# A mixture-of-experts kernel: the loads of an expert's weights issued one block later on ACT, with flags for the blocks around in the table of experts

## The chip, the cores and the metric

The kernel runs on one core of a Trainium2 chip. The time is the device time of one execution in microseconds, and lower is better. Five engines work side by side, each with an instruction queue of its own: PE (matrix products), ACT and DVE (element-wise work), POOL (here mostly gathers and scatters by index) and SP (here only DMAs). They wait for each other by semaphores.

## The reference

Three stages follow each other. Shapes: q, k, v and alpha are 4 x 8 x 768 x 48, which gives 3072 tokens of 384 features.

```python
for t in range(S):                       # gated linear attention
    state = alpha[:, :, t, :, None] * state + einsum('bhd,bhe->bhde', k[:, :, t], v[:, :, t])
    y[:, :, t] = einsum('bhd,bhde->bhe', q[:, :, t], state)
# mixture of 8 experts, one per token: w1 is (8, 384, 1024), w2 is (8, 1024, 384)
expert_idx = argmax(normalised(x) @ normalised(expert_emb).T / tau, axis=1)
for e in range(8):
    mask = expert_idx == e
    h = maximum(x[mask] @ w1[e], 0.0)
    out[mask] = gate_w[mask, None] * (h @ w2[e])
# last network: w_in is (384, 2048), w_out is (2048, 384)
h = x @ w_in
return maximum(0.01 * h, h) @ w_out
```

## The kernel before

Products are made in parts: each fp32 operand is split into a rounded part, which ACT writes, and the rest, which DVE gets by subtracting that from the original; three products of parts replace one. So every weight is loaded as fp32 into `raw`, rounded by ACT (`split_hi`, L409) and subtracted by DVE (`split_lo`, L415) into `wts`. `wts` has two sets; expert e uses set e & 1. `raw` has a half for w1 and a half for w2, each 1.5 MB, which takes three DMAs (`load_half`, L423), three roundings and three subtractions ("pieces"). A half of `raw` can be loaded again once DVE has subtracted its three pieces, for which `load_half` waits on its engine (`w_lo[half]`).

The experts' stage (about 137 to 450 us of the execution) works on 31 windows of 128 tokens, sorted by expert, at most one expert a window. The table `wtab` holds for each window its expert and a flag for the first window of an expert. With these inputs experts 0 to 7 have 4, 3, 3, 4, 4, 3, 3 and 7 windows (the last are partly empty), so windows 0, 4, 7, 10, 14, 18, 21 and 24 are first ones.

Each engine runs `step(w, u)` for w = 0 to 30, u being w's parity. In order:

- PE: x·w1 of window w + 2 (`block_hidden`, L1519, 18 matmuls), in an odd window with the transposes of h of window w between its halves (`turn_h`, L1530); the transposes of the rows of window w + 3 (`turn_gx`, L1495); then h·w2 of window w (`contract`, L1539, 24 matmuls).
- ACT: the two halves of h of window w rounded into `hT` (`h_round`: L816 from PSUM in odd windows, L820 from `hds` in even ones); relu of window w + 2 (L805, L810); the rounding of the rows of window w + 3 (`gx_round`, L799); if w + 2 is the first window of an expert, the next expert's w1 rounded and then the w1 after that loaded (`first_weights`); if w is a first window, the same with w2 (`second_weights`).
- DVE: the rests of these, in the same order (L1268 or L1271 for hT, L1142 for the rows, L415 for the weights), and last the copy of window w's result out of PSUM (L1315), for which the next contraction and POOL's scatter wait.
- In even windows h is turned by DVE in 32 x 32 squares (L1261) and SP moves the squares to their place by 16 small DMAs (`move_h`, L531, hds<-hs), for which ACT's L820 waits. POOL gathers the rows of window w + 4 (L652).

The order on each engine is written by hand; windows 4 to 27 or so are the body of a hardware loop, of two windows. ACT's part of the step that is concerned ends so:

```python
if ahead(w, 2):
    e, first = follower(act, w + 2)
    with act.If(first > 0):
        first_weights(w + 2, e)
e, first = follower(act, w)
with act.If(first > 0):
    second_weights(w, e)
```

Of the kernel before, what the change touches and what calls it, by code (L numbers as in the profile page):

```python
# [24 lines left out]
def build(nc, qka, v, emb, tau, weights, x_dram, y_dram, gate_dram, out):  # L25
# [9 lines left out]
    E, F = weights.shape[0] - 2, 1024  # L35
# [39 lines left out]
    with ExitStack() as ctx:  # L75
# [307 lines left out]
        def table(eng, w):  # L383

            return eng.value_load(wtab[0:1, ds(w, 1)], min_val=0, max_val=2 * E - 1)  # L385
# [45 lines left out]
        def next_expert(eng, e):  # L431
            return e + 1 if isinstance(e, int) else eng.snap(e + 1)

        def follower(eng, w):

            code = table(eng, w)
            return eng.snap((code & (E - 1)) + 1), eng.snap(code & E)
# [269 lines left out]
        def _(act):  # L707
# [145 lines left out]
            def step(w, u):  # L853
                if isinstance(w, int) and w == 0:

                    e, first = follower(act, 1)
                    with act.If(first > 0):
                        first_weights(0, 1)
                        first_weights(1, e)
# [5 lines left out]
                    with act.If(act.snap(E - first) > 0):  # L865
# [14 lines left out]
                with act.If(first > 0):  # L880
                    second_weights(w, e)
# [10 lines left out]
            each_window(act, step)  # L892
# [44 lines left out]
        def _(dve):  # L937
# [217 lines left out]
            start("main", dve.scalar_tensor_tensor(out=code, in0=first, scalar=float(E), in1=expert, op0=ALU.mult, op1=ALU.add))  # L1155
            after("main")
# [117 lines left out]
            def step(w, u):  # L1274
                if isinstance(w, int) and w == 0:
                    e, first = follower(dve, 1)
                    with dve.If(first > 0):
                        split_lo(dve, 1, 1, W1_PIECES)
                        split_lo(dve, e, next_set(dve, e), W1_PIECES)
                    gx_rest(2, 0)  # L1280
                    place_slots()
                for half in range(2):
                    h_rest(w, u, half)
                if isinstance(w, int) and w == 0:
                    with dve.If(dve.snap(E - first) > 0):
                        split_lo(dve, 1, 1, W1_PIECES)
# [8 lines left out]
                if ahead(w, 2):  # L1295
                    e, first = follower(dve, w + 2)
                    with dve.If(first > 0):
                        split_lo(dve, e, next_set(dve, e), W1_PIECES)
                e, first = follower(dve, w)
                with dve.If(first > 0):  # L1300
                    split_lo(dve, e, next_set(dve, e), W2_PIECES)
# [405 lines left out]
```

## Time and profile before

| | |
|---|---|
| median of 3 runs | 851.62 us (851.6 to 852.6) |
| the profiled execution's own time | 852.63 us |
| its span in the profile | 850.9 us |
| PE busy | 819.3 us, 96% of the span |
| PE weight loads, DVE, ACT, POOL busy | 86%, 51%, 40%, 24% |
| mean granted clock of PE | 0.996 |
| chain that ended last | PE 80%, DVE 5%, issue 5%, ACTq 3%, ACT 3% |

The profiled execution is the slowest of the three. Its span leaves out 1.7 us of the time. The busy share of PE is that of matmuls that overlap, so that it says little of what could be gained; the waits ahead of its matmuls say more.

### The profile page before, as it was taken

To read this page: it belongs to the slowest core of one execution; us is meant where nothing else is said; L and a number is where in the kernel's file an instruction comes from. 1 tells how busy PE (TensorE), PEld (TensorE's weight loads), DVE (VectorE), ACT (ScalarE), POOL (GpSimd) and SP (SyncE) were. 2 spreads that over 40 slices of the span, in tenths; PEclk is the share of its full clock that TensorE was granted. 3 is DMA by queue.
4 is the path that set the end of the run, shared out by engine and by line. 5 is a ranking of instruction groups with operands and counts; after the bars stand their busy time and mean duration, and the time that the engine had idled before them with its cause. 6 is when DMAs were issued, how large, how long until landed. Compare 5 with 4: busy or idle time off the path is not lost.

```text
span 850.9 us, 17254 instructions
## 1 busy us (share of the span) xinstructions
PE 819.3 (96%) x5379; PEld 734.0 (86%) x5380; DVE 434.1 (51%) x672; ACT 341.9 (40%) x643; POOL 200.0 (24%) x279
## 2 busy tenths in 40 slices
PE   7999999899989999899999999999999999999998
PEld 6888887788878888788998998998998988898997
DVE  7899986656455454455265433533433443343332
ACT  2555564444344443444253323333333333333233
POOL 6667613122233222323124003003002001000100
PEclk9999999999999999999999999999999999999999
DMA  9988665644464446647303201201011000000101
GB/s 222 268 250 245 190 205 183 204 137 129 134 219 142 142 140 169 216 158 190 101 4 41 38 1 38 37 1 37 6 32 37 1 0 18 19 1 0 38 1 38
DMA packets 55384, 85.83 MB, mean 101 GB/s; under 512 B 26855, under 2 KB 40723, under 8 KB 55344
## 3 DMA queue, kind: packets, MB, share of 16 engines
q1 hardware_dynamic: 39248, 45.24, 19.9%
q10 hardware_dynamic: 10208, 25.23, 9.0%
q0 software_dynamic: 5888, 14.85, 5.3%
q8 instruction: 22, 0.36, 0.2%
q14 instruction: 18, 0.15, 0.1%
HBM read 63.69 MB, written 15.64 MB: 93 GB/s over the span
## 4 chain that ended last, share of the span: by engine, by line
PE 80%; DVE 5%; issue 5%; ACTq 3%; ACT 3%; DMA 1%; POOL 1%; DVEq 0%; SPq 0%; POOLq 0%
PE bank L1566 24%; PE bank L1611 24%; PE bank L1539 11%; PE bank L1519 9%; PE bank L1361 2%; PE bank L1401 2%; DVE wts L415 2%; PE bank L1378 2%; ACT wts L409 2%; ACTq L423 2%; PE bank L1409 1%; PE bank L1367 1%; PE bank L1530 1%; ACTq L385 1%; PE bank L1421 1%
## 5 line engine op out<-in xcount | busy, mean ns | idle before, releaser
L1566 PE MATMUL bank<-yT,wts 128*128 128x512 f32 x864 | 217.3, 395 | 0.9 <-DVE ys L1315 0.9
L1611 PE MATMUL bank<-wts,gs 128*128 128x384 f32 x1152 | 215.4, 335 | 0.4 <-ACT os L910 0.2
L1611 PEld LDWEIGHTS bank<-wts,gs 128*128 128x128 f32 x1152 | 202.2, 188 | 10.6 <-issue 1.6
L1566 PEld LDWEIGHTS bank<-yT,wts 128*128 128x128 f32 x864 | 160.6, 188 | 31.9 <-issue 1.2
L1185 DVE TENSOR_TENSOR g<-bank,small 128x512 f32<-128x512 f32 x96 | 66.4, 691 | 175.7 <-ACT small L847 175.7
L1539 PE MATMUL bank<-wts,hT 128*128 x744 | 138.5, 341 | 17.0 <-DVE hT L1268 8.7
L1539 PEld LDWEIGHTS bank<-wts,hT 128*128 128x128 f32 x744 | 129.6, 190 | 20.7 <-issue 20.5
L1519 PE MATMUL bank<-wts,gxT 128*128 (+1 forms) x549 | 134.9, 395 | 1.3 <-DVE gxT L1142 1.3
L847 ACT ACTIVATE small<-bank 128x512 f32<-128x512 f32 x96 | 57.6, 600 | 186.5 <-PE bank L1566 186.0
L1519 PEld LDWEIGHTS bank<-wts,gxT 128*128 128x128 f32 x549 | 101.3, 188 | 20.8 <-issue 1.6
L1328 DVE TENSOR_TENSOR gs<-g,gs 128x512 fp32r<-128x512 f32 x96 | 66.5, 693 | 66.4 <-ACT gs L921 66.4
L921 ACT ACTIVATE gs<-g 128x512 fp32r<-128x512 f32 x96 | 60.7, 632 | 77.6 <-DVE g L1185 74.6
L701 POOL DMA_INDIRECT out<-os,tokens x20 | 19.7, 986 | 288.1 <-ACT os L910 283.5
L415 DVE TENSOR_TENSOR wts<-raw,wts 128x1024 f32 (+1 forms) x60 | 70.2, 1220 | 21.4 <-ACT wts L409 20.9
L678 POOL DMA_INDIRECT y_rows<-ys,idst x31 | 33.5, 1081 | 201.3 <-DVE ys L1315 193.6
L409 ACT ACTIVATE wts<-raw 128x1024 f32 (+1 forms) x60 | 59.5, 1055 | 11.2 <-issue 10.8
L816 ACT ACTIVATE hT<-bank 128x512 fp32r<-128x512 f32 x34 | 18.5, 595 | 66.4 <-issue 37.3
L820 ACT ACTIVATE hT<-hds 128x512 fp32r<-128x512 f32 x28 | 16.1, 624 | 57.7 <-DMA hds<-hs 21.6
L1315 DVE COPY ys<-bank 128x384 f32<-128x384 f32 x31 | 17.1, 553 | 43.1 <-PE bank L1539 43.1
L1268 DVE TENSOR_TENSOR hT<-bank,hT 128x512 fp32r<-128x512 f32 x34 | 21.9, 685 | 33.5 <-ACT hT L816 33.5
L652 POOL DMA_INDIRECT xg<-x_rows,isrc x27 | 29.6, 1095 | 23.8 <-POOL isrc L647 23.8
L605 POOL TENSOR_TENSOR qt<-qkas,decay 112x512 f32<-112x512 f32 x24 | 30.7, 1280 | 17.5 <-DVE decay L960 17.5
(174 smaller groups left out, 762.6 us busy)
## 6 DMA issues: line engine op xcount, KB each, us to landing
raw<-weights ACTq DMA_DIRECT2D x48, 512.0 KB
qkas<-qka SPq DMA_DIRECT2D x20, 675.5 KB, 5.7
hds<-hs SPq DMA_DIRECT2D x224, 32.0 KB
raw<-weights SPq DMA_DIRECT2D x12, 512.0 KB
vs<-v SPq DMA_DIRECT2D x24, 192.0 KB, 4.6
x_rows<-xs SPq DMA_DIRECT2D x24, 192.0 KB, 3.8
yl<-y_rows SPq DMA_DIRECT2D x20, 192.0 KB, 5.1
qkas<-qka SPq DMA_DIRECT2D x4, 227.5 KB, 6.8
```

What stands on the lines that cost most here:

```text
L409: act.activation(set_of(par, 0, cols), raw[:, cols], ACT.Copy).then_inc(w_hi[j // 3], 1)
L415: dve.tensor_tensor(set_of(par, 1, cols), raw[:, cols], set_of(par, 0, cols).bitcast(F32), ALU.subtract).then_inc(w_lo[j // 3], 1)
L605: pool.tensor_tensor(qt[0:PW, b], q_in[b][0:PW], decay[0:PW, b], ALU.mult).then_inc(qt_ready, 1)
L678: pool.indirect_dma_start(out=y_dram, out_offset=bass.IndirectOffsetOnAxis(ap=idst[:, u:u + 1].bitcast(U32), axis=0), in_=ys[:, u, :], in_ ...
L847: act.activation(small[:, f % 2], gps[f % 2][:, :], ACT.Copy, scale=0.01).then_inc(small_done, 1)
L921: act.activation(gs[:, f % 4, 0], g[:, f % 2], ACT.Copy).then_inc(g_hi, 1)
L1185: dve.tensor_tensor(g[:, f % 2], gps[f % 2][:, :], small[:, f % 2], ALU.max).then_inc(g_done, 1)
L1328: dve.tensor_tensor(gs[:, f % 4, 1], g[:, f % 2], gs[:, f % 4, 0].bitcast(F32), ALU.subtract).then_inc(g_lo, 1)
L1519: m = pe.matmul(hps[u][half][:, :], gxT[:, u, x_part, k * P:(k + 1) * P], set_of(par, w_part, slice(n, n + HALF)), start=(k == 0 and (x_pa ...
L1539: m = pe.matmul(yeps, hT[:, h_part, k * P:(k + 1) * P], set_of(par, w_part, slice(n, n + D)), start=(k == 0 and (h_part, w_part) == (0, 0) ...
L1566: m = pe.matmul(gps[f % 2][:, :], wts[:, 0, w_part, n:n + P], yT[:, 1 - u, y_part, k], start=(k == 0 and (w_part, y_part) == (0, 0)), stop ...
L1611: m = pe.matmul(ops[tt], gs[:, f % 4, g_part, tt * P:(tt + 1) * P], wts[:, 1, w_part, f * D:(f + 1) * D], start=(f == 0 and (g_part, w_par ...
```

## The change

`load_half` leaves `first_weights` and `second_weights`. ACT now issues the load of w1 in the window after that of the roundings which it follows, and that of w2 likewise, right behind `gx_round`. To know when, the table gets three more flags per window (is w + 1, w + 2 or w - 1 the first window of an expert), made by three more operations of DVE, and ACT and DVE read the table at the head of each step (`experts`), ACT once more for each load. The roundings of expert 1's w2 move from window 0 to window 1, and the load behind them to window 2. ACT's windows 2 and 3 are written out ahead of the loop. PE's, POOL's and SP's programs stay.

The diff, ACT's step first, then DVE's table and, last, DVE's step:

```diff
-        def follower(eng, w):
+        def experts(eng, w):
             code = table(eng, w)
-            return eng.snap((code & (E - 1)) + 1), eng.snap(code & E)
+            return eng.snap(code & (E - 1)), *(eng.snap(code & (E << j)) for j in range(4))
...
             def first_weights(s, e):
                 wait_from(act, h_ready, s * 2)
                 split_hi(act, e, next_set(act, e), W1_PIECES)
-                load_half(act, 0, next_expert(act, e))
 
             def second_weights(w, e):
                 act.wait_ge(ye_ready, w + 1)
                 split_hi(act, e, next_set(act, e), W2_PIECES)
-                load_half(act, 1, next_expert(act, e))
...
             def step(w, u):
+                e, first, first1, first2, first_front = experts(act, w)
...
                 if ahead(w, 3):
                     gx_round(w + 3, 1 - u)
+
+                if isinstance(w, int) and w == 0:
+                    with act.If(act.snap(2 * E - first1) > 0):
+                        load_half(act, 0, 2)
+                if ahead(w, 1):
+                    with act.If(first1 > 0):
+                        load_half(act, 0, act.snap((table(act, w + 1) & (E - 1)) + 2))
+                if isinstance(w, int) and w == 1:
+                    with act.If(first > 0):
+                        load_half(act, 1, 2)
+                elif isinstance(w, int) and w == 2:
+                    load_half(act, 1, act.snap((table(act, w - 1) & (E - 1)) + 2))
+                elif not (isinstance(w, int) and w == 0):
+                    with act.If(first_front > 0):
+                        load_half(act, 1, act.snap((table(act, w - 1) & (E - 1)) + 2))
                 if ahead(w, 2):
-                    e, first = follower(act, w + 2)
+                    with act.If(first2 > 0):
+                        first_weights(w + 2, act.snap(e + first1 // (2 * E) + 2))
+                if isinstance(w, int) and w == 0:
+                    with act.If(first1 > 0):
+                        second_weights(0, 1)
+                elif isinstance(w, int) and w == 1:
+                    second_weights(1, act.snap(e + 1))
+                else:
                     with act.If(first > 0):
-                        first_weights(w + 2, e)
-                e, first = follower(act, w)
-                with act.If(first > 0):
-                    second_weights(w, e)
+                        second_weights(w, act.snap(e + 1))
...
-            each_window(act, step)
+            each_window(act, step, apart=2)
...
             start("main", dve.scalar_tensor_tensor(out=code, in0=first, scalar=float(E), in1=expert, op0=ALU.mult, op1=ALU.add))
+            for j, by in enumerate((1, 2, -1)):
+                to, at = slice(max(-by, 0), W - max(by, 0)), slice(max(by, 0), W - max(-by, 0))
+                after("main")
+                start("main", dve.scalar_tensor_tensor(out=code[:, to], in0=first[:, at], scalar=float(2 * E << j),
+                                                       in1=code[:, to], op0=ALU.mult, op1=ALU.add))
...
             def step(w, u):
+                e, first, first1, first2, _ = experts(dve, w)
...
+                elif isinstance(w, int) and w == 1:
+                    e1 = dve.snap(e + 1)
+                    split_lo(dve, e1, next_set(dve, e1), W2_PIECES)
```

On ACT, in the loop's even window, the roundings of w1 and what stands behind them, before (ISA and REGISTER_ALU are register work, `w1_lo` is DVE's count of subtracted pieces):

```order
L409 ACTIVATE wts<-raw 128x1024
L409 ISA
L409 ACTIVATE wts<-raw 128x1024
L420 ISA
L423 ISA [waits w1_lo]
L423 DMA raw<-weights 128x1024
L423 ISA
L423 DMA raw<-weights 128x1024
L423 ISA
L423 DMA raw<-weights 128x1024
L877 UNCONDITIONAL_BRANCH
```

And in the changed kernel, at the same place:

```order
L409 ACTIVATE wts<-raw 128x1024
L409 ISA
L409 ACTIVATE wts<-raw 128x1024
L888 UNCONDITIONAL_BRANCH
L896 REGISTER_ALU
L896 COMPARE_AND_BRANCH
```

The wait and the three DMAs have gone from behind the roundings. They now stand in the same window ahead of them, behind the rounding of the rows, under a branch of their own:

```order
L797 ACTIVATE gxT<-bank 128x384 [waits gx_turned]
L877 REGISTER_ALU
L877 COMPARE_AND_BRANCH
L385 ISA
L385 TENSOR_LOAD wtab
L385 ISA x2
L420 REGISTER_ALU
L420 ISA
L423 ISA [waits w1_lo]
L423 DMA raw<-weights 128x1024
L423 ISA
L423 DMA raw<-weights 128x1024
```

On DVE, at the end of an even window and the start of the odd one, before:

```order
L399 UNCONDITIONAL_BRANCH [waits scattered0]
L1315 COPY ys<-bank 128x384 [waits ye_ready]
L1266 ISA
L1268 TENSOR_TENSOR hT<-bank,hT 128x512 [waits ht_hi]
L1266 REGISTER_ALU
```

and now:

```order
L399 UNCONDITIONAL_BRANCH [waits scattered0]
L1346 COPY ys<-bank 128x384 [waits ye_ready]
L385 ISA
L385 TENSOR_LOAD wtab
L385 ISA x2
L1290 ISA
L1292 TENSOR_TENSOR hT<-bank,hT 128x512 [waits ht_hi]
```

The read of the table has moved between the copy and the first subtraction of the next window; it stood behind the rows' subtraction (L1142), twice a window.

## Rows read from the trace of the kernel before

**Rows 1.** Chain of waits, 151 to 437 us: total, times, longest.

```profile
ACT hT L816 <- issue: 37.3, 9, 5.4
...
ACT hT L820 <- DMA hds<-hs: 21.6, 5, 5.8
...
ACT hT L820 <- issue: 17.8, 4, 4.9
...
PE bank L1539 <- DVE hT L1268: 8.7, 7, 2.1
...
PE bank L1539 <- DVE hT L1271: 6.7, 4, 2.1
```

**Rows 2.** Timeline of PE: matmuls with w2 (start, duration, idle before them).

```profile
151.35 4.44 PE L1539 MATMUL bank<-wts,hT 128*128 x24
...
265.96 4.45 PE L1539 MATMUL bank<-wts,hT 128*128 x24 [0.97 <-DVE hT L1268]
...
274.62 4.40 PE L1539 MATMUL bank<-wts,hT 128*128 x24
...
411.33 4.40 PE L1539 MATMUL bank<-wts,hT 128*128 x24
...
420.84 4.43 PE L1539 MATMUL bank<-wts,hT 128*128 x24
```

**Rows 3.** Timeline, window 12: roundings of w1, loads and what follows.

```profile
276.03 2.96 ACT L409 ACTIVATE wts<-raw 128x1024 f32 x3 [0.47 <-issue]
277.35 3.50 DVE L415 TENSOR_TENSOR wts<-raw,wts 128x1024 f32 x3 [0.99 <-ACT wts L409]
...
281.01 1.36 ACTq L423 DMA_DIRECT2D raw<-weights  x3
...
283.32 1.09 ACT L816 ACTIVATE hT<-bank 128x512 fp32r<-128x512 f32 x2 [4.34 <-issue]
...
285.01 1.31 PE L1539 MATMUL bank<-wts,hT 128*128 x6 [0.63 <-issue]
```

**Rows 4.** Timeline, window 27, which has no weights.

```profile
418.29 1.09 ACT L816 ACTIVATE hT<-bank 128x512 fp32r<-128x512 f32 x2 [6.02 <-PE bank L1530]
...
418.92 1.29 DVE L1268 TENSOR_TENSOR hT<-bank,hT 128x512 fp32r<-128x512 f32 x2 [2.59 <-ACT hT L816]
```

**Rows 5.** Timeline, start of the windows: PE, and DVE's cover for the table.

```profile
144.92 0.56 DVE L1142 TENSOR_TENSOR gxT<-bank,gxT 128x384 fp32r<-128x384 f32 x1 [1.65 <-ACT gxT L799]
...
157.11 2.35 PE L1519 MATMUL bank<-wts,gxT 128*128 x9 [1.32 <-DVE gxT L1142]
...
164.77 5.97 PE L1539 MATMUL bank<-wts,hT 128*128 x24 [2.05 <-DVE hT L1268]
```

**Rows 6.** Windows of 1 us: ..., granted clock, DMA share, GB/s.

```profile
165.00:166.00 1.00, 1.00 (x4) 1.00 (x5) 0.43 (x2) 0.98 (x3) 1.00 (x1) 0.50 1.04 375
```

**Rows 7.** Timeline, window 5: DVE's subtractions and what follows.

```profile
208.06 3.50 DVE L415 TENSOR_TENSOR wts<-raw,wts 128x1024 f32 x3 [0.74 <-ACT wts L409]
...
211.47 0.55 DVE L1315 COPY ys<-bank 128x384 f32<-128x384 f32 x1
...
216.18 1.14 PE L1539 MATMUL bank<-wts,hT 128*128 x5 [1.28 <-DVE hT L1271]
```

**Rows 8.** Line L385, 273 to 296 us: reads of the table, ns min/median/max.

```profile
L385 DVEq TENSOR_LOAD <-wtab x6: 301/308/364, 275.7 to 295.7; - x6
```

**Rows 9.** Timeline, window 12: moves of hs and the gather.

```profile
274.06 10.08 SPq L531 DMA_DIRECT2D hds<-hs  x16
...
274.38 1.05 POOL L652 DMA_INDIRECT xg<-x_rows,isrc  x1 [0.88 <-POOL isrc L647]
```

**Rows 10.** Tile xg, whole execution: gathers from issue to landing.

```profile
DMA to landing us min/median/max: 3.1/4.6/6.5
```

**Rows 11.** Windows of 2 us around a load: ..., clock, DMA share, GB/s.

```profile
283.00:285.00 2.00, 1.37 (x8) 0.93 (x6) 1.04 (x2) 1.68 (x4) 1.11 (x3) 1.00 0.96 367
...
289.00:291.00 2.00, 2.00 (x11) 1.70 (x10) 1.42 (x3) 1.16 (x2) 0.07 (x1) 1.00 0.00 0
```

More of the change, by code:

```diff
@@ L383, in table @@
         def table(eng, w):
-            return eng.value_load(wtab[0:1, ds(w, 1)], min_val=0, max_val=2 * E - 1)
+            return eng.value_load(wtab[0:1, ds(w, 1)], min_val=0, max_val=16 * E - 1)
         def set_of(par, part, cols):
@@ L853, in step @@
             def step(w, u):
+                e, first, first1, first2, first_front = experts(act, w)
                 if isinstance(w, int) and w == 0:
-                    e, first = follower(act, 1)
-                    with act.If(first > 0):
+                    with act.If(first1 > 0):
                         first_weights(0, 1)
-                        first_weights(1, e)
+                        load_half(act, 0, 2)
+                        first_weights(1, 2)
                     relu(1, 1, 0)
@@ L864, in step @@
                     h_round(0, 0, 1)
-                    with act.If(act.snap(E - first) > 0):
+                    with act.If(act.snap(2 * E - first1) > 0):
                         first_weights(0, 1)
@@ L874, in step @@
                     gx_round(w + 3, 1 - u)
-                if ahead(w, 2):
-                    e, first = follower(act, w + 2)
+                if isinstance(w, int) and w == 0:
+                    with act.If(act.snap(2 * E - first1) > 0):
+                        load_half(act, 0, 2)
+                if ahead(w, 1):
[9 more added lines that the diff above has]
+                        load_half(act, 1, act.snap((table(act, w - 1) & (E - 1)) + 2))
+                if ahead(w, 2):
+                    with act.If(first2 > 0):
+                        first_weights(w + 2, act.snap(e + first1 // (2 * E) + 2))
+                if isinstance(w, int) and w == 0:
+                    with act.If(first1 > 0):
+                        second_weights(0, 1)
+                elif isinstance(w, int) and w == 1:
+                    second_weights(1, act.snap(e + 1))
+                else:
                     with act.If(first > 0):
-                        first_weights(w + 2, e)
-                e, first = follower(act, w)
-                with act.If(first > 0):
-                    second_weights(w, e)
+                        second_weights(w, act.snap(e + 1))
+                if not ahead(w, 1):
+                    with act.If(first > 0):
+                        load_half(act, 1, SET_OUT)
                 if isinstance(w, int) and w == 1:
@@ L1274, in step @@
             def step(w, u):
+                e, first, first1, first2, _ = experts(dve, w)
                 if isinstance(w, int) and w == 0:
-                    e, first = follower(dve, 1)
-                    with dve.If(first > 0):
+                    with dve.If(first1 > 0):
                         split_lo(dve, 1, 1, W1_PIECES)
-                        split_lo(dve, e, next_set(dve, e), W1_PIECES)
+                        split_lo(dve, 2, 0, W1_PIECES)
                     gx_rest(2, 0)
@@ L1284, in step @@
                 if isinstance(w, int) and w == 0:
-                    with dve.If(dve.snap(E - first) > 0):
+                    with dve.If(dve.snap(2 * E - first1) > 0):
                         split_lo(dve, 1, 1, W1_PIECES)
@@ L1295, in step @@
                 if ahead(w, 2):
-                    e, first = follower(dve, w + 2)
+                    with dve.If(first2 > 0):
+                        e2 = dve.snap(e + first1 // (2 * E) + 2)
+                        split_lo(dve, e2, next_set(dve, e2), W1_PIECES)
+                if isinstance(w, int) and w == 0:
+                    with dve.If(first1 > 0):
+                        split_lo(dve, 1, 1, W2_PIECES)
+                elif isinstance(w, int) and w == 1:
+                    e1 = dve.snap(e + 1)
+                    split_lo(dve, e1, next_set(dve, e1), W2_PIECES)
+                else:
                     with dve.If(first > 0):
[L1298 to L1301, printed above, removed]
+                        e1 = dve.snap(e + 1)
+                        split_lo(dve, e1, next_set(dve, e1), W2_PIECES)
                 if isinstance(w, int) and w == WINDOWS - 3:
```

2 lines of the change are left out of this document (removed).

## Prediction

> **What bounds it now.** I read the chain of waits for the experts' stage first, then the timeline of PE, then that of all engines around the places where PE waits. The chain shows 15.4 us (8.7 + 6.7) in 11 waits of PE's contractions for DVE's part of `hT`; and on ACT 13 waits put down to "issue" ahead of the very roundings of `hT` on which DVE depends, 37.3 us in nine and 17.8 us in four [rows 1]. Issue means that nothing in the data held ACT: its own queue did.
>
> Window 12 shows how. ACT's three roundings end at 278.99. DVE's three subtractions follow and end at 280.85. Only then come the three DMAs (281.01 to 282.37), and the rounding of window 13's h starts at 283.32; contraction 13 waits 0.63 us for it [rows 3]. Window 27, with no weights, is the contrast: ACT's rounding starts 6.96 us after contraction 26, when PE's transposes are there, and DVE's 0.63 us later [rows 2, 4]. In window 12 the rounding came 8.70 us after its contraction [rows 2, 3].
>
> How much is there in all? The waits undercount it, since they begin at modelled ends of matmuls, so I use the distances between contractions [rows 2]. Undisturbed, even to odd takes 9.51 us (411.33 to 420.84) and odd to even 8.66 (265.96 to 274.62), a pair 18.17. From window 0 to 26 are 13 pairs: 236.2 us; the trace has 411.33 - 151.35 = 259.98. So 23.8 us are lost between windows 0 and 26. Behind them no weights are loaded by this code, and the last network runs at PE's own pace, so a gain up to there reaches the end whole.
>
> **What the change does.** (a) *The wait leaves ACT's path.* A load has 1.86 us of waiting for DVE (278.99 to 280.85) and 1.5 us of issue behind its roundings [rows 3]; both go. Sixteen loads are ACT's; all late contractions of windows 1 to 25 stand behind one. Without them ACT's rounding in an odd window is set by PE's transposes, as in window 27, in time for the contraction [rows 4].
>
> (b) *The load is issued a window later, ahead of any roundings there.* It waits for nothing, DVE being long done, but costs ACT 1.36 us for the DMAs and about 0.7 for a branch and a table read (0.3 a read on either engine [rows 8], the rest register work; estimate): 2.1 us. With no roundings in that window it lies in time in which ACT has nothing to do, since the next even rounding can't start before the contraction's end, 4.4 us after its start [rows 2]. With roundings behind it, they start at 1.41 (276.03 - 274.62 [rows 2, 3]) + 2.1 = 3.5 us after the contraction's start. That is so in windows 5, 8, 19 and 22, where an expert of three windows puts both together.
>
> (c) *There DVE becomes the last.* First rounding done at 3.5 + 1.0, subtractions 3.5 us, copy about 0.5 net, then the table read that now stands between copy and subtraction, and the first half of h's rest: 4.5 + 3.5 + 0.5 + 0.4 + 0.7 = 9.6 us [rows 3, 4, 7, 8]. In windows 5 and 19 the next contraction is due at 8.66: 1.0 us of wait each, against 1.28 in window 6 now [rows 7]. In 8 and 22 it is due at 9.51: 0.1 to 0.2 each. Sum 2.3. Bounds: nothing, if table read and copy overlap and the load costs ACT 1.4; 5 us, if each of the four costs a microsecond more than that.
>
> (d) *Roundings alone* (seven windows with w2, two with w1): 1.4 + 1.0 + 3.5 + 0.5 + 0.4 + 0.7 = 7.5 us, before 8.66 and 9.51: no wait left. If the table reads cost 1.2 us more than I think, the odd ones of these (7 and 21) would wait; nothing in the rows asks for that.
>
> (e) *The start.* Window 0 loses the wait of ACT behind the first roundings, so that `gx_round` comes at once; PE waited 1.32 us for it and 2.05 us ahead of contraction 1 [rows 5]. The roundings of expert 1's w2 go to window 1, beside the shifted logits and the exponential: contraction 2 is then DVE's to delay, by between 0 and 2.05 us (the row of the same sort [rows 5]); from DVE's list I take 0.5, and 0.3 for window 3, behind the load of window 2. Contraction 1 took 5.97 us instead of 4.4 [rows 2, 5]: PE had stood still before it, and the granted clock is 0.50, 1.2 GHz, in that stretch [rows 6]. With both idle times gone I expect the dip to go, worth 1.5 us, which is inside the 23.8.
>
> (f) *Three operations of DVE for the flags*: under a microsecond in all, behind which DVE waited 1.65 us for ACT [rows 5]: nothing; without that cover 0.7.
>
> (g) *Where the transfers go.* A load issued at 281.01 keeps the DMA engines near 1.0 at 283 to 285 and is gone by 289 [rows 3, 11]: some 7 us. hs's squares take SP 10.1 us to issue, from 0.6 us ahead of the even contraction [rows 2, 9], and are due some 16.9 us after it (18.17 less roundings). Five waits for them stand on ACT now, 21.6 us [rows 1], since loads come 6.4 us after the contraction and end last. In the changed kernel a load comes 1.2 us or 10.5 us after it; the first ends before the squares do, the second begins when they are in. The gather of rows goes out 0.24 us before a contraction and is due 8.7 us or more later; the slowest landing is 6.5 [rows 2, 9, 10]. It now meets the load sooner; cover 2.2 us. I count nothing.
>
> Sum: of the 23.8 us, 2.3 stay by (c) and 0.5 + 0.3 by (e), so **20.7 us** go. Against the profiled execution 852.6 - 20.7 = 831.9; the median of the runs is 1.0 below the profiled one, so 830.9.
>
> **Rivals.**
>
> *A, the forecast*: ACT freed, small waits for DVE left, 831; with the bounds of (c) and (e) 828.5 to 835.
>
> *B, another engine takes over most of it*: DVE's chain at every rounding, or the squares of hs. For: DVE is the releaser in all 11 named waits, and copies stand behind its subtractions. Against: in window 5 DVE had finished its copy at 212.02, and contraction 6 came at 216.18 [rows 7]. If each of 16 places kept 0.7 us: 852.6 - 1.0 - 23.8 + 11 = 839; 835 to 845.
>
> *C, late data.* The Trainium skill ("DMA: Bandwidth & Descriptors", Rules for kernel authors) says to issue a DMA early and wait for it late; the change issues later. As a mechanism here: the piece isn't in `raw` when ACT wants to round it, and ACT stands with h's rounding behind. The shortest way from issue to use is two windows less, 18.17 us, for a transfer of some 7 [rows 2, 3, 11]; it decides only if transfers took 11 us more. At 1 us for each of 15, 846. By that page the kernel would lose; no row speaks for it.
>
> *D, slower than before*: a load right behind `gx_round` meets the gather, so that PE waits for rows. The same skill page (Issuing engines are not separate DMA queues) says that all queues share the 16 engines. The gather must land over 8.7 us after issue, and over 10.0 us at all 16 loads to eat the 20.7 us (1.3 each); then 852 and more. Against it: 6.5 us is the most in a trace where loads met gathers already [rows 10].
>
> *E, nothing*: the waits were covered by others, 851.6. Window 27 speaks against it [rows 4].
>
> **Chances.** A 0.70, B 0.16 (all faster), C 0.04 (faster still), D 0.04, E 0.02; 0.04 for a gain of 23 us or more. Under 0.2% (1.7 us) a measurement of this kernel can't tell from no change. Faster 0.94, same 0.02, slower 0.04. Range 828 to 839: A with its bounds and B's better half.
>
> **What would show it.** In the changed profile: PE's waits for L1292 and L1295 (the old L1268 and L1271) fall from 15.4 to about 4 us, the largest ahead of contractions 6 and 20; "issue" ahead of ACT's roundings of hT is gone in odd windows; contractions 0 to 26 take about 239.3 us; no clock of 0.5 in window 1; waits of ACT for hds are nearly gone. If contractions after rounding windows still start 0.5 us late or more everywhere, (d) is wrong; if PE waits for xg, (g) is.

## The result and the profile after

The changed kernel takes 841.87 us (median of 4 runs, 841.5 to 842.52), the kernel before 851.81 in the same comparison (4 runs, 851.6 to 852.6): a ratio of 0.9882, interval 0.9865 to 0.990. It is faster, by 9.9 us instead of 20.7, and lies outside the forecast range of 828 to 839. Two later comparisons gave 0.9865 (0.9837 to 0.9894) and 0.9856 (0.9838 to 0.9874).

The profiled execution took 841.64 us (span 839.9), 10.99 less than that of before. First the timeline of PE in it, the contractions 0, 1, 2, 26 and 27 (L1570 was L1539), which answers to [rows 2]:

```profile
153.15 4.40 PE L1570 MATMUL bank<-wts,hT 128*128 x24
162.65 4.43 PE L1570 MATMUL bank<-wts,hT 128*128 x24
171.48 4.45 PE L1570 MATMUL bank<-wts,hT 128*128 x24
...
400.35 4.41 PE L1570 MATMUL bank<-wts,hT 128*128 x24
409.88 4.43 PE L1570 MATMUL bank<-wts,hT 128*128 x24
```

Contractions 0 to 26 take 400.35 - 153.15 = 247.20 us: 12.8 less than before, 7.9 more than the 239.3 forecast, 11.0 above PE's own 236.2. The first contraction is 1.8 us later than in the trace of before, and from contraction 26 to the end both take 439.55. So 12.8 - 1.8 = 11.0, the whole difference.

What PE waits for between 153 and 401 us, by the view of waits (total, times, longest):

```profile
PE bank L1570 <- issue: 3.4, 5, 0.8
PE bank L1526 <- DMA xg<-x_rows,isrc: 2.2, 2, 1.2
PE bank L1570 <- DVE hT L1295: 1.5, 2, 0.8
PE bank L1570 <- DVE hT L1292: 0.7, 2, 0.4
```

And of ACT's waits between 140 and 440 us, all that stand ahead of the roundings of hT:

```profile
ACT hT L814 <- PE bank L1561: 49.0, 14, 7.1
...
ACT hT L818 <- PE bank L1570: 36.8, 11, 4.7
```

Against [rows 1]: ACT's "issue" and its waits for `hds` are gone, and it waits only for PE, which costs nothing. PE's waits for DVE fell from 15.4 to 2.2 us. New is what the prediction named as the sign of a failed step (g): PE's transposes of the rows (L1526) wait for the gather `xg`, and five contractions wait for "issue" with no other name.

I take the distance of each contraction from the one before and subtract 9.51 us (even to odd) or 8.66 (odd to even). The losses stand in two groups. Contractions 6, 9, 20 and 23 lose 1.01, 0.63, 0.99 and 0.63 (3.3 us together); these follow the windows with a load ahead of roundings. Contractions 3, 7, 10, 21 and 24 lose 2.26, 1.21, 0.71, 0.97 and 2.41 (7.6 us): the place and the sort are new.

The chain of what ended last, around contraction 3 (start, us, what):

```profile
173.70 8.16 DMA xg<-x_rows,isrc
181.86 0.04 issue
181.91 0.55 PE bank L1526 x3
182.46 0.80 issue
183.25 0.79 PE bank L1570 x3
```

The gather starts at 173.70, 2.22 us behind contraction 2, and not 0.24 us ahead of it as in window 12 of before [rows 2, 9]. It lands after 8.2 us, where 6.5 was the most before [rows 10]. PE then does its transposes and needs 0.80 us more to start the contraction.

Why the gather is late shows in the timeline of windows 5 and 6, all engines:

```profile
201.43 4.43 PE L1570 MATMUL bank<-wts,hT 128*128 x24
...
202.91 1.35 ACTq L423 DMA_DIRECT2D raw<-weights  x3
...
204.87 2.96 ACT L409 ACTIVATE wts<-raw 128x1024 f32 x3 [2.51 <-issue]
...
206.18 3.50 DVE L415 TENSOR_TENSOR wts<-raw,wts 128x1024 f32 x3 [3.23 <-ACT wts L409]
...
209.59 0.55 DVE L1346 COPY ys<-bank 128x384 f32<-128x384 f32 x1
...
210.06 1.28 DVE L1295 TENSOR_TENSOR hT<-hds,hT 128x512 fp32r<-128x512 f32 x2
...
211.03 1.21 POOL L676 DMA_INDIRECT y_rows<-ys,idst  x1 [8.01 <-DVE ys L1346]
211.10 4.44 PE L1570 MATMUL bank<-wts,hT 128*128 x24 [0.78 <-DVE hT L1295]
...
211.39 1.35 ACTq L423 DMA_DIRECT2D raw<-weights  x3
...
213.31 1.05 POOL L650 DMA_INDIRECT xg<-x_rows,isrc  x1 [0.88 <-POOL isrc L645]
```

The load stands ahead of the roundings, so ACT rounds 3.44 us behind contraction 5, DVE subtracts up to 209.68, and only then copies the result of window 5. POOL's queue is in order: the scatter of window 5 waits 8.01 us for this copy, and behind the scatter stands the gather of window 6, which so goes out 2.21 us behind contraction 6. By then ACT has issued window 6's load (211.39), and the view of windows shows the DMA engines filling up behind it (PE, PE loads, DVE, ACT, POOL, clock, DMA share, GB/s):

```profile
212.00:214.00 2.00, 2.00 (x14) 2.00 (x13) 1.00 (x2) 0.00 (x0) 1.11 (x3) 1.00 0.70 92
214.00:216.00 2.00, 2.00 (x12) 1.91 (x12) 0.42 (x1) 0.00 (x0) 0.68 (x3) 1.00 1.00 407
216.00:218.00 2.00, 2.00 (x13) 1.66 (x12) 0.14 (x1) 0.00 (x0) 0.97 (x1) 1.00 1.04 404
```

The gather of 213.31 landed after 7.2 us. The same chain stands in windows 2, 6, 9, 20 and 23, where the gather starts 2.03 to 2.22 us behind the contraction (elsewhere at most 0.4 behind), and the next contraction loses in exactly these five. In window 2 the late copy is that of window 1, which now stands behind the roundings of expert 1's w2.

### The profile page after: what moved, and what is told of

It is laid out like the page before. It is cut to its first block, busy times and chain, and to the rows that moved or that the text cites. A ratio compares the mean times of both kernels' runs of the same rounds, so it can differ in the third digit from the quotient of the medians.

```text
span 839.9 us, 17215 instructions
## 1 busy us (share of the span) xinstructions
PE 817.0 (97%) x5379; PEld 732.0 (87%) x5380; DVE 434.3 (52%) x675; ACT 344.0 (41%) x643; POOL 198.2 (24%) x279
## 4 chain that ended last, share of the span: by engine, by line
PE 84%; DMA 5%; issue 4%; DVE 3%; ACTq 1%; ACT 1%; POOL 1%; DVEq 1%; SPq 0%; POOLq 0%
PE bank L1597 24%; PE bank L1642 24%; PE bank L1570 12%; PE bank L1550 12%; DMA qkas<-qka 2%; PE bank L1392 2%; PE bank L1432 2%; PE bank L1409 2%; DMA xg<-x_rows,isrc 2%; PE bank L1561 1%; PE bank L1440 1%; PE bank L1398 1%; PE bank L1526 1%; ACT wts L409 1%; ACTq L423 1%
## 5 line engine op out<-in xcount | busy, mean ns | idle before, releaser
L1570 PE MATMUL bank<-wts,hT 128*128 x744 | 137.0, 338 | 5.7 <-issue 3.4
L1570 PEld LDWEIGHTS bank<-wts,hT 128*128 128x128 f32 x744 | 128.3, 188 | 8.2 <-issue 8.0
L650 POOL DMA_INDIRECT xg<-x_rows,isrc x27 | 28.4, 1052 | 23.8 <-POOL isrc L645 23.8
L979 DVE TENSOR_TENSOR_SCAN decay<-qkas,bank 112x512 f32<-112x512 f32 x24 | 29.2, 1216 | 5.9 <-ACT bank L717 4.9
L608 POOL TENSOR_TENSOR kt<-qkas,inv 112x512 f32<-112x512 f32 x24 | 30.8, 1284 | 5.2 <-DVE inv L987 4.0
```

The lines of the kernel that those rows point to most:

```text
L608: pool.tensor_tensor(kt[0:PW, b % 2], k_in[b][0:PW], inv[0:PW, b % 2], ALU.mult).then_inc(kt_ready, 1)
L1570: m = pe.matmul(yeps, hT[:, h_part, k * P:(k + 1) * P], set_of(par, w_part, slice(n, n + D)), start=(k == 0 and (h_part, w_part) == (0, 0) ...
```

## The experiments

Theory 1 is this chain: a late copy on DVE holds POOL's scatter, that holds the gather, the gather meets a load and lands late. In these experiments a "stage" is the time from contraction 0 to 26. The comparisons were made in three groups, each beside the kernel before (853.21, 851.53 and 852.17 us). The results first:

Losses of 0.1 us and less are left out of the sums. Where PE's first contraction starts differs between the profiles by up to 4.6 us, for a reason that lies ahead of the windows (see "What stays open"); so the stage compares two versions better than the time does.

| version | time, us | ratio (interval) | stage | lost ahead of 3, 7, 10, 21, 24 | ahead of 6, 9, 20, 23 |
|---|---|---|---|---|---|
| changed kernel, first | 841.87 | 0.9882 (0.9865 to 0.990) | 247.20 | 7.6 | 3.3 |
| x1 load behind | 828.27 | 0.9717 (0.969 to 0.9743) | 236.81 | 0.6 | 0 |
| x2 gather early | 832.48 | 0.977 (0.974 to 0.9801) | 241.45 | 0.2 | 4.6 |
| x3 both | 828.92 | 0.9724 (0.97 to 0.9747) | 237.31 | 0 | 0 |
| x4 DVE read back | 840.36 | 0.9866 (0.9833 to 0.9898) | 246.27 | 5.7 | 3.3 |
| y0 changed kernel | 839.65 | 0.9865 (0.9837 to 0.9894) | 246.16 | 6.5 | 3.3 |
| y1 short loads | 833.38 | 0.9784 (0.9761 to 0.9808) | 240.99 | 1.3 | 3.1 |
| y2 before, gather early | 851.99 | 0.9996 (0.9978 to 1.0014) | 260.52 | as before | as before |
| y3 second w2 in window 0 | 839.15 | 0.9851 (0.9828 to 0.9875) | 246.51 | 5.3 | 3.3 |
| z0 changed kernel | 840.2 | 0.9856 (0.9838 to 0.9874) | 247.63 | 8.1 | 3.1 |
| z1 load behind | 829.35 | 0.9726 (0.9713 to 0.9739) | 237.30 | 1.1 | 0 |
| z2 load behind, w2 in 0 | 828.08 | 0.9716 (0.9698 to 0.9734) | 236.28 | 0 | 0 |

**x1: the load of w2 behind the roundings of w1.** One block of ACT's step, the roundings of w1, moves up between the load of w1 and that of w2 (`...` stands for the branches of windows 1 and 2):

```diff
                     with act.If(first1 > 0):
                         load_half(act, 0, act.snap((table(act, w + 1) & (E - 1)) + 2))
+                if ahead(w, 2):
+                    with act.If(first2 > 0):
+                        first_weights(w + 2, act.snap(e + first1 // (2 * E) + 2))
...
                     with act.If(first_front > 0):
                         load_half(act, 1, act.snap((table(act, w - 1) & (E - 1)) + 2))
-                if ahead(w, 2):
-                    with act.If(first2 > 0):
-                        first_weights(w + 2, act.snap(e + first1 // (2 * E) + 2))
```

> The changed kernel with the load of w2 behind the roundings of w1 where both fall in one window (2, 5, 8, 19, 22), nothing else moved. Theory 1 (a late chain): in these windows ACT's load pushes roundings and DVE's subtractions back, so DVE's copy of the window's result is late, so POOL's scatter and the gather behind it are late, the gather meets the next window's load, and PE waits for rows. Then both kinds of loss go: contractions 0 to 26 take 237.5 to 239.5 us instead of 247.2, and the time is some 833.5 us. Theory 2 (loads slow the gathers wherever they stand): only DVE's direct delays of contractions 6, 9, 20 and 23 go, 3.3 us in all: 838.6 us. Theory 3 (the table read at the head of DVE's step is what costs): DVE's copy is earlier but the read stays: 841 us.

828.27 us, and both groups of losses go, but for 0.64 us ahead of contraction 3: the copy of window 1 still stands behind roundings, and the gather of window 2 still starts 2.22 us behind contraction 2. The timeline of window 5 in x1:

```profile
196.47 4.43 PE L1570 MATMUL bank<-wts,hT 128*128 x24
...
197.57 2.01 ACT L409 ACTIVATE wts<-raw 128x1024 f32 x2 [0.16 <-issue]
...
198.78 0.86 ACTq L423 DMA_DIRECT2D raw<-weights  x2
198.88 3.50 DVE L415 TENSOR_TENSOR wts<-raw,wts 128x1024 f32 x3 [0.88 <-ACT wts L409]
...
202.29 0.55 DVE L1346 COPY ys<-bank 128x384 f32<-128x384 f32 x1
...
205.12 1.98 PE L1570 MATMUL bank<-wts,hT 128*128 x10
...
206.02 1.05 POOL L650 DMA_INDIRECT xg<-x_rows,isrc  x1 [0.88 <-POOL isrc L645]
```

The first rounding comes 1.10 us behind the contraction instead of 3.44, the copy 5.82 instead of 8.16, contraction 6 comes on time (8.65), and the gather 0.90 us behind it instead of 2.21. The load's three issues still come in this window: they stand behind the roundings in ACT's program and go out while the last two of these are computed, so they delay nothing. Of the 5 us by which the time came out below my number, 3.3 are an earlier contraction 0 (149.84), which this edit doesn't explain (below); the stage was 236.81 for 237.5 to 239.5.

**x2: the gather in front of the scatter**, one window further ahead; the roundings and the load stay as changed.

```diff
-                if ahead(w, 4):
-                    pool.wait_ge(gx_turned, w + 3)
-                    copy_index(w * 3 + 1, isrc, slot_src, w + 4, u)
-                    gather(u, isrc[:, u:u + 1])
+                if ahead(w, 5):
+                    pool.wait_ge(gx_turned, w + 4)
+                    copy_index(w * 3 + 1, isrc, slot_src, w + 5, 1 - u)
+                    gather(1 - u, isrc[:, 1 - u:2 - u])
                 wait_scattered(pool, w, u, pool_turns)
```

> The changed kernel with POOL's gather of window w + 5 ahead of the scatter of window w, so that no gather waits for DVE's copy. Theories 1 and 2: the waits for rows and PE's slow restart behind them go (contractions 3, 7, 10, 21, 24: 7.6 us over the undisturbed distance), DVE's direct delays of 3.4 us stay: 834.3 us. Theory 3: no change, 841.9 us.

Only the gather losses go (0.2 of 7.6 are left); contractions 9, 20 and 23 lose what they lost. DVE, ACT and the loads do what they did, so the late gathers alone were those 7.4 us. The time is below the 834.3 expected although the stage, 241.45, is 1.9 above what this theory leaves of it (236.2 + 3.4): contraction 0 was 3.5 us earlier than in the changed kernel. Contraction 6 lost 2.48 us here, 1.5 more than in the changed kernel, and the trace shows where: the load that ACT issues ahead of the roundings took twice its time in this execution.

```profile
197.82 2.72 ACTq L423 DMA_DIRECT2D raw<-weights  x3
...
201.15 2.96 ACT L409 ACTIVATE wts<-raw 128x1024 f32 x3 [3.98 <-issue]
```

Why it took 2.72 us and not 1.35 is open. It shows that the price of issues ahead of roundings isn't a fixed one.

**x3: both edits.**

> The changed kernel with both edits (load of w2 behind the roundings of w1, gather ahead of the scatter). Theory 1: nothing but 0.2 us ahead of contraction 2 is left of the 11.0 us that contractions 0 to 26 lose: 831 us. Theory 2 the same, since the gather has 13 us to land. If this is not under 833, something else holds windows that no theory names.

828.92 us, the same as x1 within the intervals; its one loss over 0.2 us, 0.8, is ahead of contraction 4. That it is 2 us under the 831 expected is again the early contraction 0 (148.58). With the copies on time the early gather has nothing to add.

**x4: DVE reads the table behind the rests of hT and of the rows**, and not at the head of the step.

```diff
             def step(w, u):
-                e, first, first1, first2, _ = experts(dve, w)
...
+                if not (isinstance(w, int) and w == 0):
+                    e, first, first1, first2, _ = experts(dve, w)
                 if ahead(w, 2):
                     with dve.If(first2 > 0):
```

> The changed kernel with DVE's read of the table put back behind the subtraction of the rows' rest, as before the change, so that none stands between the copy and the next subtraction. Theory 3: the direct delays (3.4 us) go and with them most of what follows: 833 to 836 us. Theory 1: the read's 0.5 us in five windows, the copy is as late as it was: 839.5 to 841.5 us.

The stage is 246.27, between 246.16 and 247.63 of the changed kernel's three profiles: the place of this read is worth nothing that shows. The view of L385 says why: in the changed kernel DVE's queue reads the table from 209.1 us on, for 0.30 us, while the last subtraction runs (up to 209.68), and L1295 starts 0.47 us behind the start of the copy, with the read or without it (210.06 behind 209.59; in x4 206.38 behind 205.92). The four losses ahead of 6, 9, 20 and 23 stay as well (1.11, 0.62, 1.00 and 0.60). At the start the losses moved: contraction 2 lost 0.81 us for 0.17, and contraction 3 1.17 for 2.26.

**y0: the changed kernel again.**

> The changed kernel itself, timed once more beside the others and profiled again. Two things are open. First, the stage of windows: contractions 0 to 26 took 247.20 us in the first profile, with 7.6 us lost ahead of contractions 3, 7, 10, 21 and 24 (the late gathers) and 3.3 us ahead of 6, 9, 20 and 23 (the roundings behind a load). If these come from the order of the work, the second profile repeats them within some tenths: 246.3 to 248, and a time of 841 to 843. If the collision of gather and load is a matter of chance, single losses appear and go, and the stage moves by more than 2 us. Second, contraction 0 started at 153.15 us in the first profile, 1.8 us later than in that of the kernel before and 3.4 us later than in two of the versions tried since, whose code ahead of it differs in nothing that runs there. If that is the chip's doing (a dip of the clock in the attention stage), it starts anywhere from 148.5 to 153.2 again; if it belongs to the change, at 153 again.

The losses are at the same nine contractions, so they belong to the order of the work; each of the four that make up the 3.3 us repeats within 0.02, while those behind a gather vary (1.81 against 2.41 ahead of contraction 24). Contraction 0 starts at 152.73.

**y1: loads of an eighth of the columns**, which takes the traffic away and leaves the order and the waits.

```diff
+                n_cols = PC if eng is nc.sync else PC // 8
-                eng.dma_start(raw[:, (half * 3 + j) * PC:(half * 3 + j + 1) * PC],
-                              src[:, j * PC:(j + 1) * PC]).then_inc(raw_in[half], 16)
+                eng.dma_start(raw[:, (half * 3 + j) * PC:(half * 3 + j) * PC + n_cols],
+                              src[:, j * PC:j * PC + n_cols]).then_inc(raw_in[half], 16)
```

> The changed kernel with ACT's loads of weights cut to an eighth of their columns, so that the products of experts 2 to 7 are made with stale weights; the issue of the loads, the waits and the roundings stay. Theory 1 (DVE's copy is late behind a load on ACT, so POOL's scatter and gather are late, and the gather then meets the next window's load): the gather goes out as late as before, but lands in 4 to 5 us instead of 8, which is inside the 6.3 us that are left to PE's transposes; the losses ahead of contractions 3, 7, 10, 21 and 24 (7.6 us) go, those ahead of 6, 9, 20 and 23 (3.3 us, issue and DVE) stay. Contractions 0 to 26 take 239.5 to 240.3, the time is 833.5 to 835.5. Rival 1a (the gather is late by POOL alone, whatever else is on the queues): the losses stay, stage 246 to 247.5, time 841 to 843. Rival 1b (the issue of a load costs ACT what it does since the transfers push back on it, as in the 2.72 us that one load took in a version with early gathers): 6, 9, 20 and 23 shrink as well, stage 237 to 238, time 831 to 832.

The gathers start as late as before (2.04 to 2.23 us behind contractions 2, 3, 6, 9, 20 and 23), and those of windows 2, 6, 9 and 20 land after 3.4, 3.4, 3.4 and 3.3 us, where the changed kernel had 8.2, 7.2, 6.0 and 7.0. The view of the tile `xg` in y1, over all gathers:

```profile
DMA to landing us min/median/max: 3.1/3.4/6.4
```

The losses behind these four are gone (0.23 us is left ahead of contraction 3); those of the other group stay. So it takes both, the late start and the load. Rival 1a falls, 1b too. The fifth, ahead of contraction 24, keeps 1.10 us (and so the stage is 0.7 us above the 240.3 expected): in window 23 SP reads results back for the last network right ahead of the gather.

```profile
364.96 1.91 SPq L551 DMA_DIRECT2D yl<-y_rows  x4
365.25 1.42 ACTq L424 DMA_DIRECT2D raw<-weights  x3
...
366.54 1.06 POOL L651 DMA_INDIRECT xg<-x_rows,isrc  x1 [0.88 <-issue]
```

This gather landed in 6.4 us. Other large transfers than the loads of weights may do the same, then; that these reads do was not tried apart.

**y2: the gather early in the kernel before**, POOL's edit of x2.

> The kernel before, with POOL's gather of rows sent one window ahead and in front of the scatter, as in the version of the changed kernel in which the gather losses were gone. Theory 1: in the kernel before no contraction waits for rows (its gathers go out 0.24 us before a contraction and land in 6.5 us at most), so nothing changes: ratio 0.998 to 1.002, contractions 0 to 26 take 259.5 to 260.5. Rival 2 (early gathers help by themselves, since the copy, the scatter and the gather share POOL with other work that PE waits for): 2 us or more faster here too.

0.9996: an early gather is worth nothing where the copy is on time. Rival 2 falls.

**y3: the second w2 rounded in window 0 again.**

```diff
                 if isinstance(w, int) and w == 0:
-                    with act.If(first1 > 0):
-                        second_weights(0, 1)
-                elif isinstance(w, int) and w == 1:
-                    second_weights(1, act.snap(e + 1))
+                    second_weights(0, 1)
                 else:
                     with act.If(first > 0):
                         second_weights(w, act.snap(e + 1))
```

> The changed kernel with one part undone: expert 1's w2 is rounded in window 0 again and not in window 1; its load stays in window 2. My step (e) put the move of these roundings and of the load behind them among the causes of the 2.05 us wait ahead of contraction 1 and of the clock dip behind it (3.9 us lost in window 1 before, nothing in the changed kernel). If the roundings in window 0 are the cause: contraction 1 is lost by 1.5 to 4 us again, the time is 843.5 to 846. If the wait of ACT and the loads were the cause and the roundings have room in window 0: contraction 1 on time, contraction 2 loses nothing, the time 841.5 to 842.2. The loss ahead of contraction 3 (2.26 us), which theory 1 puts on the load of window 2, stays in both cases.

Contraction 1 is on time (151.47 to 161.01 us, with the three roundings between them), so window 0 has room for them. What made it late before stood behind them. The timeline of before, ahead of contraction 1 (164.77 [rows 5]):

```profile
161.66 1.39 ACTq L423 DMA_DIRECT2D raw<-weights  x3
163.10 1.08 ACT L816 ACTIVATE hT<-bank 128x512 fp32r<-128x512 f32 x2 [4.04 <-issue]
```

Without the wait and the DMAs ACT rounds h at 158.46 here. But I was wrong on contraction 3. Its loss went from 2.26 to 0.21, since the copy of window 1 isn't behind roundings any more, and contractions 4 and 10 lost 1.67 and 1.68 instead (10 had lost 0.6 to 1.0 in the changed kernel's profiles; here its gather took 7.0 us to land and not 6.0, and why is open). In window 3 the gather now started 2.05 us behind the contraction: that of window 2, whose roundings stand behind a load. Undoing the part moved the late gather of the start by one window, and the loss ahead of 10 grew; so it was worth nothing.

**z0, z1 and z2**: the changed kernel and x1 once more in one group, and x1 with the edit of y3.

> The changed kernel once more, beside the version below. Contraction 0 has started at 153.15 and 152.73 us in its two profiles, and at 148.6 to 149.8 in four versions that ran in one other job. If the start is set by the job (the chip or its memory), both kernels of this job start alike; if by the layout of the code, the changed kernel starts at 152.7 to 153.2 again and the version with the load behind at 149.8. Its stage of windows takes 246 to 247.5 us in any case.

> The changed kernel with the load of w2 behind the roundings of w1, a second time: contractions 0 to 26 take 236.5 to 237.2, as in its first profile (236.81), and the time is 827 to 831, by where contraction 0 starts. Its ratio to the kernel before lies at 0.970 to 0.976. If the first result owed its last 3 us to a lucky start, the time comes out at 830 to 831.5 with contraction 0 at 151 to 153.

> The version with the load behind, and expert 1's w2 rounded in window 0 again. In the changed kernel this move back was worth nothing (839.15 against 839.65), since losses came back in other windows. Theory 1: with the load behind nothing is late, and both are at PE's pace, so the time is that of the version with the load behind within 1 us, contractions 0 to 26 at 236.2 to 237.5. Rival 2: the roundings in window 0 delay POOL's first scatters as a load ahead did in window 2, and contraction 3 or 4 waits for rows: 1 to 2 us lost.

z1 repeats x1 (829.35), 10.85 us below z0, of which the stage makes 247.63 - 237.30 = 10.3. Its own loss is 1.06 us ahead of contraction 3. z2 loses nothing at all: its stage of 236.28 us is PE's own 236.2. It is the best version here by its median, 828.08 us, ratio 0.9716; z1's interval touches it, so the two are not told apart by time. Both beat the kernel before by 23 to 24 us and the changed one by 11 to 12.

The traces together also give the price of a late gather. Gathers that PE waited for (of those whose landing a trace gives; window, start behind its contraction, landing after the start, loss of the next contraction):

| window, version | start | landing | loss | landing - loss |
|---|---|---|---|---|
| 2, changed kernel | 2.22 | 8.16 | 2.26 | 5.90 |
| 2, y0 | 2.22 | 8.06 | 2.17 | 5.89 |
| 2, z0 | 2.23 | 8.11 | 2.22 | 5.89 |
| 2, z1 | 2.23 | 7.0 | 1.06 | 5.9 |
| 6, changed kernel | 2.21 | 7.2 | 1.21 | 6.0 |
| 20, changed kernel | 2.21 | 7.0 | 0.97 | 6.0 |
| 3, y3 | 2.05 | 6.9 | 1.67 | 5.2 |
| 9, changed kernel | 2.03 | 6.0 | 0.71 | 5.3 |
| 9, y3 | 2.04 | 7.0 | 1.68 | 5.3 |
| 23, changed kernel | 2.03 | 7.71 | 2.41 | 5.30 |
| 23, y0 | 2.04 | 7.11 | 1.81 | 5.30 |
| 23, z0 | 2.04 | 8.44 | 3.14 | 5.30 |
| 23, y1 | 2.04 | 6.4 | 1.10 | 5.3 |
| 23, x4 | 2.04 | 7.3 | 1.99 | 5.3 |
| 23, y3 | 2.04 | 7.4 | 2.10 | 5.3 |

The last column is constant within 0.1 us for each parity: what a gather lands later than 5.9 us (even) or 5.3 us (odd) behind such a start is lost one for one. Since the next contraction is due 9.51 - 2.22 = 7.29 us behind the even start and 8.66 - 2.03 = 6.63 behind the odd one, the rows must be there 1.4 or 1.3 us ahead of it. That is the 0.55 of the transposes and the 0.80 of issue in the chain above.

## Why the prediction was wrong, by its own steps

**(a) held.** ACT's waits for DVE and its issue behind roundings are off the path. In z2 nearly all of the 23.8 us that it found in the distances of contractions came back (259.98 - 236.28 = 23.7): the size was real.

**(b) held, as to time.** First rounding 3.44 us behind contraction 5, for 3.5. In window 8 the three issues took 1.75 us instead of 1.36, and the rounding came at 3.9.

**(c) held in its mechanism, a size was off.** The working gave contraction 6 at 9.6 us behind contraction 5, and it came at 9.67. Part of that closeness is luck: the 0.4 us for the table read aren't on the path (x4), and between the end of the first half of h's rest (210.74) and the contraction (211.10) lie 0.36 us that the working left out. Contractions 6 and 20 lost 1.01 and 0.99, for 1.0 each; 9 and 23 lost 0.63 each, for 0.1 to 0.2. The term was 3.3 and not 2.3: 1.0 us short. What 9 and 23 lost above the forecast is what the roundings of windows 8 and 22 started later than that of window 5 (3.91 us behind the contraction for 3.44), 0.4 of it in the issue of the load. The upper bound was added up wrongly, too: a microsecond more at each of four contractions makes 2.3 + 4 = 6.3 us, and not 5.

**(d) held** for the contraction right behind: none that follows roundings alone lost over 0.2 us. What it left out was the copy, below.

**(e) held for what it looked at.** Contraction 2 lost 0.17 for 0.5, contraction 1 nothing, and the dip in window 1 is gone: the mean granted clock from 30 to 839 us is 1.00. The view of windows, where [rows 6] had 0.50:

```profile
165.00:166.00 1.00, 1.00 (x8) 1.00 (x7) 0.90 (x4) 1.00 (x3) 0.00 (x0) 1.00 0.14 37
```

For contraction 3 it said 0.3, on account of DVE, and 2.26 came, on account of the gather. By y3 and x1, that took the roundings in window 1 and the load of window 2 together: without the first 0.21 is left, with the load moved back 0.6 to 1.1.

**(f) held.** The three operations take 0.64 us, and DVE still waits 1.55 us for ACT some time behind them, where it waited 1.65 before [rows 5]:

```profile
139.73 0.64 DVE L1178 SCALAR_TENSOR_TENSOR wflag<-wflag 128x30 f32<-128x30 f32 x3
...
146.69 0.56 DVE L1161 TENSOR_TENSOR gxT<-bank,gxT 128x384 fp32r<-128x384 f32 x1 [1.55 <-ACT gxT L797]
```

x4 found the table read worth nothing too.

**(g) is the step that failed**: "The gather of rows goes out 0.24 us before a contraction and is due 8.7 us or more later; the slowest landing is 6.5 [...] cover 2.2 us. I count nothing." Three things in it were wrong. The start was read from window 12, and taken as fixed. It hangs on DVE's copy, by way of the scatter ahead of it in POOL's queue, and step (c) had just worked out that DVE's copy would be 2 to 3 us later in four windows; I followed that copy to PE and not to POOL. Then the cover was too large from the start: rows must be there 1.3 us ahead of the contraction, which leaves 8.66 + 0.24 - 1.33 - 6.5 = 1.1 us and not 2.2. And 6.5 us was no bound for a gather behind a load: 7 to 8.4 are seen here. With a start 2.03 to 2.22 us behind the contraction the cover for a landing of 6.5 is below zero. It cost 7.6 us, where 0.3 was forecast for contraction 3 alone. Of these, 1.1 us ahead of contraction 24 stayed in y1, where the loads move an eighth: they hang on the late start, but not on the load of weights.

**The sum**, in the profiled execution: 10.99 us gained against 20.7. Of the 9.7 between them 7.3 are (g), with the 0.3 of (e) taken off, and 1.0 are (c); 0.3 are given back by contraction 2; and 1.8 are the later contraction 0, which no step had, and which y1, y3, z1 and z2, with the same code ahead of the windows, don't have (below). (With two digits, 7.26 + 0.96 - 0.33 + 1.80 = 9.69.)

**The rivals.** D had the mechanism, a load that meets the gather, and I gave it 0.04 because I priced it only as a case in which all 16 loads do it, so that it decided the sign. At five places it costs a third of the gain. A rival that decides the sign and the same mechanism as a partial loss are two different cases, and the second had no chance in my list, nor a place in the range. The Trainium skill ("DMA: Bandwidth & Descriptors", Issuing engines are not separate DMA queues) says that DMAs from all engines interleave on the same 16; the trace agrees, the share being at 1.00 while the gather of 213.31 is under way, and in y1, with loads of an eighth, the same gather lands after 3.4 us and not 7.2. B's range, 835 to 845, held the time of all three comparisons (841.87, 839.65 and 840.2), but not for its reason: PE's waits for DVE are 2.2 us. C and E fell: no rounding waited for `raw`.

**What stays open.** Contraction 0 started at 153.15, 152.73 and 152.38 us in the three profiles of the changed kernel, at 151.35 and 152.22 in two of before (y2 among them), at 148.6 to 149.8 in x1 to x4, and at 151.0 to 151.5 in y1, y3, z1 and z2. x1 and z1 are the same code, 1.2 us apart, and z0 and z1 ran beside each other, 1.4 apart. Neither the group of the comparison nor the layout of the code explains it alone. The traces do sort them, by where in the attention stage one stretch of some 3.4 us has a granted clock of 0.50, the lower level of 1.2 GHz:

| low stretch | contraction 0 starts | versions |
|---|---|---|
| none | 148.6 to 149.8 | x1, x2, x3, x4 |
| between 13 and 18 us | 151.0 to 151.5 | before, y1, y3, z1, z2 |
| between 25 and 29 us | 152.4 to 153.2 | changed kernel, y0, z0 |
| 49.8 to 53.2 us | 152.2 | y2 |

So x1 and z1 differ as the first two rows do, and z0 and z1 as the second and the third. And the 1.8 us between the traces of before and of the changed kernel are there before 41 us, long ahead of the code that was changed: the 401st matmul starts at 38.50 us in the one and at 40.37 in the other. Half the clock for 3.4 us can cost PE at most 1.7 us, so it is not all of the difference between the first and the third row. The view of windows of before, and then of the changed kernel:

```profile
15.00:18.00 3.00, 3.00 (x34) 2.90 (x30) 2.40 (x4) 1.24 (x3) 1.80 (x2) 0.51 1.06 263
26.00:28.00 2.00, 1.47 (x34) 1.26 (x30) 2.00 (x4) 1.83 (x6) 1.41 (x2) 1.00 1.11 248
```

```profile
15.00:18.00 3.00, 3.00 (x49) 2.70 (x44) 2.93 (x6) 1.12 (x3) 2.24 (x4) 1.00 1.07 244
26.00:28.00 2.00, 2.00 (x23) 1.89 (x24) 0.92 (x2) 0.48 (x2) 1.09 (x1) 0.50 1.04 248
```

PE had idled shortly before both stretches: 2.17 us ahead of the products of 12.67 us in before, 1.62 us ahead of those of 23.53 in the changed kernel. But in x2 it idled 2.01 us ahead of 12.62 us, and no stretch at the lower level followed. Why it falls at the one or the other, or not at all, was not tried. It is no part of what the change does in the windows, but a profile of one execution carries some 2 us of it either way.

## What to carry to other kernels

When an instruction gets later, follow every engine that waits for it, and on each of them what stands behind the waiting instruction in its queue. Here a copy that PE had in time held a scatter, the scatter held a gather, and the gather was what PE missed. The cover of a transfer is counted from the start that it will have after the change to the moment at which its reader's queue must go on, not to the reader's next large piece of work. And DMA issues belong behind the work that others wait for, also on an engine that seems idle: moving the three of a load behind three roundings, in five windows, was worth 11 us here.

## What the runs showed of the hardware

- A gather of 128 rows by index that lands in 3.4 to 4.6 us by the median of each version took 6.0 to 8.4 us in windows 2, 3, 6, 9, 20 and 23, where it started 0.2 to 2 us behind the first issue of a load of 1.5 MB. With loads of an eighth those of windows 2, 3, 6, 9 and 20 took 3.3 to 3.4, and that of window 23, behind SP's reads of results, 6.4. A gather 7 us behind a load and such reads took 7.2 and 7.3 us too (window 24 in z1 and z2), but as it had started ahead of its contraction, nothing was lost.
- PE needed 1.3 to 1.4 us from the landing of late rows to the first matmul of the contraction behind the three transposes: 0.55 for these, and 0.5 to 0.8 put down to issue, though the contraction's part of `hT` from DVE had been there for 1.6 us or more.
- Three DMA issues on ACT took 1.35 us mostly, 1.65 to 1.76 in four windows of the changed kernel and 2.72 once.
- DVE's queue read the table while its last subtraction was still running, so that a read of 0.30 us in front of the next subtraction cost nothing (x4).
